# Expert loop of a mixture-of-experts stage: experts written out, counts read one expert ahead, and a tile's rows taken later

## The reference, cut to what matters

```python
x = attention(q, k, v, beta)              # (3072, 384), a delta-rule scan
x = leaky_relu(x @ moe_w_in) @ moe_w_out  # (3072, 384), dense
do_compute = x @ w_skip > 0               # rows that fail this are copied
e_idx, gate_w = best of 8 experts by softmax(x @ w_gate)
for e in range(8):
    rows = do_compute & (e_idx == e)
    h = maximum(x[rows] @ w1[e], 0)             # 384 -> 1024
    out[rows] = x[rows] + gate_w * (h @ w2[e])  # 1024 -> 384
```

## Time and profile before

| | |
|---|---|
| median of 3 runs | 902.17 us (901.98 to 902.83) |
| the profiled execution | 900.34 us |
| its span, first to last instruction | 898.6 us |
| granted TensorE clock, mean | 0.968 |
| PE busy | 776.0 us, 86% |
| DVE busy | 662.2 us, 74% |
| ACT busy | 496.4 us, 55% |
| POOL busy | 414.3 us, 46% |

### The profile page before, as it was taken

One profiled execution on the slowest core, in us unless ns is written; L12 is line 12 of the kernel. 1 busy time (PEld: TensorE's weight loads), 2 busy tenths in 40 slices (PEclk: granted clock), 3 DMA queues, 4 the chain that ended last, 5 costly groups with the idle time before them and its releaser, 6 DMA issues.

```text
span 898.6 us, 27698 instructions
## 1 busy us (share of the span) xinstructions
PE 776.0 (86%) x10782; PEld 625.4 (70%) x10783; DVE 662.2 (74%) x1334; ACT 496.4 (55%) x1108; POOL 414.3 (46%) x498
## 2 busy tenths in 40 slices
PE   0122679999999999999999999999999899999996
PEld 0122558787778787777878788878777777778774
DVE  6655978888887988887888887876768873563382
ACT  5426456767666666667676756554455651441261
POOL 5104153636354544535362724352352665564463
PEclk9995589999999999999999999999999999999998
DMA  9599177687687686868667686347416765263100
GB/s 214 148 233 163 28 116 123 133 140 143 116 149 133 120 162 113 133 124 138 127 121 149 114 144 121 77 71 231 169 30 200 246 230 188 70 214 120 44 16 16
DMA packets 357277, 119.76 MB, mean 133 GB/s; under 512 B 330450, under 2 KB 348420, under 8 KB 356784
## 3 DMA queue, kind: packets, MB, share of 16 engines
q1 hardware_dynamic: 351424, 104.33, 55.7%
q0 software_dynamic: 3232, 7.64, 2.5%
q10 hardware_dynamic: 2512, 6.29, 2.0%
HBM read 63.53 MB, written 21.25 MB: 94 GB/s over the span
## 4 chain that ended last, share of the span: by engine, by line
PE 37%; DVE 20%; issue 10%; SPq 10%; DMA 8%; ACT 8%; POOL 5%; DVEq 0%; POOLq 0%; ACTq 0%
PE b_h L743 8%; PE b_acc L756 8%; PE b_acc L849 7%; PE b_h L836 6%; DVE stage L1483 3%; PE b_ch L682 3%; SPq L442 2%; DVE inv L1409 2%; SPq L498 2%; ACT operands L954 2%; DMA operands<-operands 2%; SPq L510 2%; DVE inv L1415 2%; DMA operands<-nq 1%; PE b_gr L644 1%
## 5 line engine op out<-in xcount | busy, mean ns | idle before, releaser
L1908 POOL TENSOR_TENSOR stage<-stage 128x256 f16<-128x256 f32 x192 | 143.4, 747 | 246.9 <-ACT stage L954 246.0
L743 PE MATMUL b_h<-stage,wt 128*128 128x256 f16 x1728 | 221.8, 274 | 6.7 <-DVE stage L1342 6.3
L756 PE MATMUL b_acc<-wt,stage 128*128 128x384 f16 x1152 | 218.4, 326 | 3.7 <-POOL stage L1908 2.8
L743 PEld LDWEIGHTS b_h<-stage,wt 128*128 128x128 f16 x1728 | 159.1, 98 | 27.3 <-DVE stage L1342 8.2
L756 PEld LDWEIGHTS b_acc<-wt,stage 128*128 128x128 f16 x1152 | 106.7, 97 | 58.2 <-POOL stage L1908 5.7
L954 ACT ACTIVATE stage<-stage 128x256 f16<-128x256 f32 x192 | 80.0, 417 | 108.7 <-DVE stage L1483 107.8
L1483 DVE SCALAR_TENSOR_TENSOR stage<-b_h,stage 128x256 f32<-128x256 f32 x192 | 80.7, 420 | 42.1 <-ACT stage L1074 40.4
L849 PE MATMUL b_acc<-wt,operands 128*128 128x384 f16 x552 | 98.9, 330 | 7.1 <-DVE operands L1523 7.1
L836 PEld LDWEIGHTS b_h<-y,wt 128*128 128x128 f16 x1656 | 93.5, 98 | 6.5 <-issue 4.6
L836 PE MATMUL b_h<-y,wt 128*128 128x128 f16 x1656 | 96.5, 219 | 1.5 <-DVE y L1342 0.7
L1415 DVE TENSOR_REDUCE inv<-inv 128x30 f32<-128x90 f32 (+4 forms) x180 | 84.9, 472 | 5.6
(11 more groups left out here) (215 smaller groups left out, 1293.3 us busy)
## 6 DMA issues: line engine op xcount, KB each, us to landing
operands<-in_moe_w_dram SPq DMA_DIRECT2D x18, 1536.0 KB, 7.9
a_sys<-a_dram SPq DMA_DIRECT2D x24, 256.0 KB, 4.4
kc<-operands SPq DMA_DIRECT2D x22, 256.0 KB, 4.3
natq<-in_q_dram SPq DMA_DIRECT2D x24, 192.0 KB, 4.1
raw_v<-in_v_dram SPq DMA_DIRECT2D x24, 192.0 KB, 4.2
stage<-y SPq DMA_DIRECT2D x96, 48.0 KB, 2.0
x_dram<-stage SPq DMA_DIRECT2D x24, 192.0 KB, 2.8
out_dram<-stage SPq DMA_DIRECT2D x24, 192.0 KB, 3.4
```

What stands on the lines that cost most here:

```text
L743: mm = pe.matmul(b_h[f % 2][:, 0:GT], wt[0][:, a, d * FF + f * P:d * FF + (f + 1) * P], xT[:, g % 2, b, d, :], start=(i == 0), stop=(i == ...
L756: mm = pe.matmul(b_acc[w][:, 0:DM], g16[:, f % 4, a, w * P:(w + 1) * P], wt[1][:, b, f * DM:(f + 1) * DM], start=(f == 0 and (a, b) == PAR ...
L1908: pool.tensor_tensor(g16[:, f % 4, LO, :], g32[:, f % 4, :], g16[:, f % 4, HI, :], ALU.subtract).then_inc(g_lo, 1)
```

## The change

On ACT and DVE the eight experts are written out one by one, without the loop over pairs and its `If`. The counts of expert e+1 are read after the first tile of expert e. On DVE `tile_out` of a tile moves from behind `tile_in` of the next to behind quarter 0 of the next tile, and quarter 3 moves ahead of `tile_in(t+1)`. A last `tile_out` stands at the end. On POOL the copy to `raw_v` becomes a step of its own (`keep`); from tile 3 on it stands ahead of `tile_next`. In `tile_back` two waits change places. PE and SP are as before.

```diff
@@ ScalarE @@
-            def expert(e, q, last=None):
-                n = act.value_load(tile_n[0:1, 0, ds(e, 1)], min_val=1, max_val=NT)
-                before = act.value_load(tile_n[0:1, 1, ds(e, 1)], min_val=0, max_val=FIRST + MAXT)
+            def counts(e):
+                return (act.value_load(tile_n[0:1, 0, ds(e, 1)], min_val=1, max_val=NT),
+                        act.value_load(tile_n[0:1, 1, ds(e, 1)], min_val=0, max_val=FIRST + MAXT))
+            n, before = counts(0)
+            for e in range(E):
                 act.wait_ge(eh_done, 1 + 2 * before)
                 act.sem_inc(act_waited, 1)
-                if last is None:
-                    tile(before, q)
-                else:
-                    with act.If(last < E // 2 - 1):
-                        tile(before, q)
-                    with act.If(last >= E // 2 - 1):
-                        tile(before)
+                tile(before, QUARTERS[e])
+                n_next, before_next = counts(min(e + 1, E - 1))
                 with act.If(n > 1):
                     with act.Fori(1, n) as j:
                         tile(before + j)
+                n, before = n_next, before_next
@@ VectorE @@
             tile_in(FIRST)
-            tile_out(3)
             split_lo(1, 1, 2, 2)
             def tile(t, q=(None, None, None, None)):
                 if q[0]:
                     split_lo(*q[0])
-                hidden_low(t, 0)
+                tile_out(t - 1)
                 if q[1]:
                     split_lo(*q[1])
-                hidden_low(t, 1)
+                hidden_low(t, 0)
                 if q[2]:
                     split_lo(*q[2])
-                tile_in(t + 1)
-                tile_out(t)
+                hidden_low(t, 1)
                 if q[3]:
                     split_lo(*q[3])
+                tile_in(t + 1)
...
+            n, before = counts(0)
+            for e in range(E):
+                tile(before, QUARTERS[e])
+                n_next, before_next = counts(min(e + 1, E - 1))
                 with dve.If(n > 1):
                     with dve.Fori(1, n) as j:
                         tile(before + j)
+                if e < E - 1:
+                    n, before = n_next, before_next
+            tile_out(before + (n - 1))
@@ GpSimd @@
-            def tile_back(t):
+            def keep(t):
                 pool.wait_ge(yo_ready, 1 + t)
                 waited()
                 pool.tensor_copy(xg_keep[:], tiles[:, ds(t % RING, 1), :].rearrange("p a m -> p (a m)")
                                  ).then_inc(xg_kept, 1)
+
+            def tile_back(t):
                 pool.wait_ge(yo_scattered, 16 * t + 16)
                 pool.sem_inc(yo_left, 1)
                 pool.tensor_copy(id_out[:], ids[:, ds(t, 1)]).then_inc(ids_ready, 1)
+                pool.wait_ge(ids_ready, 2 * t + 3)
+                waited()
                 pool.wait_ge(yo_ready, 1 + t + 1)
-                waited()
-                pool.wait_ge(ids_ready, 2 * t + 3)
                 waited()
...
-                tile_next(t)
+                if t < FIRST - 1:
+                    tile_next(t)
+                    keep(t)
+                else:
+                    keep(t)
+                    tile_next(t)
...
             with pool.Fori(FIRST, total) as t:
+                keep(t)
                 tile_next(t)
                 tile_back(t)
```

More of the change, by code:

```diff
@@ L1307, in _ @@
             act.wait_ge(tiles_ready, 1)
-            def expert(e, q, last=None):
-                n = act.value_load(tile_n[0:1, 0, ds(e, 1)], min_val=1, max_val=NT)
-                before = act.value_load(tile_n[0:1, 1, ds(e, 1)], min_val=0, max_val=FIRST + MAXT)
+            def counts(e):
+                return (act.value_load(tile_n[0:1, 0, ds(e, 1)], min_val=1, max_val=NT),
+                        act.value_load(tile_n[0:1, 1, ds(e, 1)], min_val=0, max_val=FIRST + MAXT))
+            QUARTERS = [((1, 1, 2, 3), None, (2, 0, 1, 0), (2, 0, 1, 1)), (None, (2, 0, 1, 2), None, (2, 0, 1, 3))]
+            QUARTERS += [[(e + 1, 1 - e % 2, e % 2, i) for i in range(4)] for e in range(2, E - 1)]
+            QUARTERS += [(None, None, None, None)]
+            n, before = counts(0)
+            for e in range(E):
                 act.wait_ge(eh_done, 1 + 2 * before)
                 act.sem_inc(act_waited, 1)
-                if last is None:
-                    tile(before, q)
-                else:
-                    with act.If(last < E // 2 - 1):
-                        tile(before, q)
-                    with act.If(last >= E // 2 - 1):
-                        tile(before)
+                tile(before, QUARTERS[e])
+                n_next, before_next = counts(min(e + 1, E - 1))
                 with act.If(n > 1):
@@ L1833, in tile, with counts @@
                     split_lo(*q[0])
-                hidden_low(t, 0)
+                tile_out(t - 1)
                 if q[1]:
                     split_lo(*q[1])
-                hidden_low(t, 1)
+                hidden_low(t, 0)
                 if q[2]:
                     split_lo(*q[2])
-                tile_in(t + 1)
-                tile_out(t)
+                hidden_low(t, 1)
                 if q[3]:
                     split_lo(*q[3])
[L1845 to L1854, removed]
+                tile_in(t + 1)
+            def counts(e):
+                return (dve.value_load(tile_n[0:1, 0, ds(e, 1)], min_val=1, max_val=NT),
+                        dve.value_load(tile_n[0:1, 1, ds(e, 1)], min_val=FIRST, max_val=FIRST + MAXT))
+            QUARTERS = [((1, 1, 2, 3), None, (2, 0, 1, 0), (2, 0, 1, 1)), (None, (2, 0, 1, 2), None, (2, 0, 1, 3))]
+            QUARTERS += [[(e + 1, 1 - e % 2, e % 2, i) for i in range(4)] for e in range(2, E - 1)]
+            QUARTERS += [(None, None, None, None)]
+            n, before = counts(0)
+            for e in range(E):
+                tile(before, QUARTERS[e])
+                n_next, before_next = counts(min(e + 1, E - 1))
                 with dve.If(n > 1):
```

## The result

The changed kernel takes 908.60 us in the median of 7 runs (905.65 to 912.88). The kernel before took 901.98 in the median of 7 beside it (899.37 to 902.89). The ratio is 1.0087, with a 95% interval of 1.0061 to 1.0113: slower by some 8 us (the two medians lie 6.6 apart). The profiled execution took 912.88, the longest of the seven, and the profiled one of before 900.34. So the two traces lie 12.5 us apart, more than half as much again as typical runs do.

A forecast was written before the change was run, and what follows sets the result against it. From 680 us on the kernel was taken as PE work with stalls in and behind weight-splitting tiles. Losses of 2.05 + 1.9 + 0.1 = 4.05 us put the profiled run at 904.4 and the median at 906.2, range 899.3 to 910.0.

The forecast's parts named there:

- the sum: Whole kernel: losses of 2.05 in quarter tiles, 1.9 by gathers and 0.1 in tile 4, together 4.05 us slower.
- Quarter tiles: Tiles that split weights: 9.14 us of DVE work ahead of the next tile bounds them; together 2.05 us lost.
- the written-out code: ACT and DVE programs: more instructions might fetch slower; taken as zero cost, at most 0.72 us.
- POOL's order: Copy to `raw_v` delays the copy to `natk` by 0.50 us; hidden in tiles without quarters.
- One more copy ahead of `natk`, 0.3: Full quarter tiles: POOL's extra copy ahead of `natk` costs PE about 0.3 us each (0 to 0.8).
- The gather behind a quarter tile: Tiles 7, 12 and 14: gathers start later and rows land late; 1.9 us lost (gain 0.6 to loss 5).
- the slower landing: Gather behind a quarter tile: landing slower by 1.3 us makes a stall of 1.9 us instead of 0.6.
- Tile 4: Earlier low half against a later gather for tile 5: 0.1 us lost, bounds gain 2.9 and loss 1.9.
- The level of the clock: Tile 4: after PE idles 2 to 3 us, tile 5 starts at 722.5 at full clock, up to 725.7 at lower.
- The inference that descriptors are written beside a DVE instruction with two SBUF inputs: Skill page's rule, doubted by the prediction; by it tile 4's issue ends some 0.8 us sooner, sum 0.8 less.
- A (faster): Rival: gathers land in time, clock stays, tile 4 gains 2.9; 2.75 us less, 899.4; chance 0.25.
- C (the gathers decide): Rival: three gathers behind weight loads cost 1.9 each, tile 4 its 1.9; 9 us slower, 911; chance 0.10.

The follow-up runs named there:

- e1: Kernel before with only experts written out and counts read one expert ahead on ACT and DVE, DVE's tile order and POOL untouched: ratio 0.9984 to the kernel before.
- e3: Kernel before with only POOL's order changed, `keep` ahead of `tile_next`: ratio 1.0015 to the kernel before.
- e5: Changed kernel with POOL's part undone, the kept copy again behind the gather: ratio 1.0084 to the kernel before.
- e9: Changed kernel with the weight loads of experts 2 to 7 bringing only an eighth of their columns: ratio 1.0013 to the kernel before.
- e12: Changed kernel with DVE's tile order as before the change and the second weight matrix's loads held back until gathered rows landed: ratio 0.9975 to the kernel before.

## Why the prediction was right, and where its sizes were off

The direction, the mechanism and the places were right; the size of one term was not. The median, 908.60, is in the stated range but just above the forecast's own 904.0 to 908.5: the loss is 6.6 us by the medians and 7.9 by the ratio, where the sum had 4.05. By the profile, of a long run, tiles 4 to 22 lost 10.5. By the steps of the prediction:

- *Quarter tiles.* Forecast: about 9.9 for tiles 11, 13 and 10.2 for 20, 10.5 for 6 and 21. Measured: 9.70, 9.89, 10.37, 10.39, 10.06. Together they lost 1.43, forecast 2.05. The 9.14 us of DVE work in a row took 9.17 in tile 11, started 0.23 after the up stage (forecast 0.3); tile 20 had 9.18 and 0.22. Tile 13 came out at its 9.9 by luck: quarter 0 started 0.43 ahead of the up stage, but one quarter took 2.72 instead of 1.75, and the row was 10.18 long. In tiles 6 and 21 it started 0.92 and 0.58 after the up stage (forecast 1.1). That the written-out code costs nothing was shown by e1, and POOL's order as a small thing by e3 and e5.
- *One more copy ahead of `natk`, 0.3.* The transposes waited 0.40 for it in tile 11 and, by the same timeline, in tiles 6, 20 and 21; without POOL's part (e5) tiles 6, 11 and 20 are 0.17 to 0.45 faster, but tile 21 is 0.41 slower.
- *The gather behind a quarter tile.* This is the mis-sized term, and by the runs nearly the whole loss: with the small loads (e9) 1.2 us of the 7.9 are left, and by its trace the quarter tiles' loss is made up by a faster tile 4. Forecast 1.9 for tiles 7, 12 and 14 together, measured 6.89. The place of the gather was right: 0.90 after the up stage in tiles 7 and 12 (forecast 0.8). The landing was put at 6.1 after the up stage and `natk` at 6.6; in tile 7 `natk` ended at 8.3 (755.27 - 746.98), in tile 12 at 7.6. The forecast took 4.3 from the issue's end to the landing; with the second matrix's load issued just ahead it was 5.8 in tile 7 and 5.1 in tile 12. That is about the slower landing that the prediction had bounded with 1.9 for each gather. The transposes waited 2.20, 1.49 and 0.88, 4.57 together. In tile 7 the clock fell as well, and its second down half took 3.79, some 1.7 more than at full clock, which no term of the sum held.
- *Tile 4.* Forecast a loss of 0.1, with a bound of 1.9 to the bad side; measured 1.83. Its rows in the changed kernel:

```profile
712.80 3.41 DVE L1338 SCALAR_TENSOR_TENSOR stage<-operands,stage 128x1536 f16<-128x1536 f32 x2
...
712.93 1.65 POOL L1943 COPY id_in<-spare 128x1 uint32<-128x1 uint32 x1 [0.17 <-POOL operands L1952]
...
715.44 1.69 POOL L1926 DMA_INDIRECT natq<-x_dram,id_in  x1 [0.85 <-POOL id_in L1943]
...
716.35 0.37 SPq L544 DMA_DIRECT2D operands<-in_moe_w_dram  x1
716.66 0.68 DVE L1519 SCALAR_TENSOR_TENSOR operands<-b_h,operands 128x512 f16<-128x512 f32 x1
...
720.13 1.78 POOL L2022 COPY raw_v<-operands 128x385 f32 x1
...
722.41 0.51 POOL L1951 COPY natk<-natq 128x384 f32<-128x384 f32 x1 [0.50 <-DMA natq<-x_dram,id_in]
```

The times after the up stage (713.18; 711.29 in the forecast) are nearly the forecast's. The copy of the row numbers got in between the two quarters and ended 1.40 after it (forecast 1.6). The gather's issue ended 3.95 after it (4.3), with SP's load of 716.35 beside it. The low half came 3.5 after it (4.0). `natk` was done 9.7 after it (8.7 to 9.6). The forecast gave all of this to the landing. But POOL's kept copy (L2022) ended only at 721.91, half a us ahead of `natk`: a quick landing would have gained that half us and no more, and e9 shows the same. The level of the clock had been left open. It fell: the second down half took 4.05 and the next up stage 4.68, some 2.4 together above the usual times. So the tile ended at the forecast's bad end, 14.32 (14.4).

The inference that descriptors are written beside a DVE instruction with two SBUF inputs, which the prediction weighed against the trace (the Trainium skill, SBUF — State Buffer, Who interferes with whom; the page names `tensor_tensor`, the instruction here is a `scalar_tensor_tensor`), fails here too: the issue at 715.44 took 1.69 with a quarter running at its start, against 1.05 for the ones alone.

Of the rivals, A (faster) fell just where it was said to decide: tile 4 took over 11 us. C (the gathers decide) is nearer to the profiled run than the forecast is, and the median of the runs lies between the two. What stays open is how the gathers vary from run to run: the changed kernel's seven runs spread over 7.2 us, those of before over 3.5, and only one of each was traced. The traced run is 4.3 us above the median, about what the low clock took in it (4.1); whether the typical run kept its clock is not shown. If it did, the terms for the gathers and tile 4 are less wrong for it than for the trace. The median is in the stated range because that range was drawn most of the way to C. That e5 and e12 moved tile 21 and tile 20 by half a us either way was not followed up.

## What to carry to other kernels

When work is moved on one engine, follow the small transfers that its neighbour issues behind it, and look what large transfer stands just ahead of them: here the rows of a gather (128 rows of 385 floats, 197 KB) were copied 6.9 us after its issue began behind a load of 1.5 MB, and 3.8 us behind a load of an eighth of that. Look also at the copies on the neighbour itself: in tile 4 they kept PE waiting 2.90 us even where the transfer was quick. A wait that holds the large load back until the small one has landed can give back most of such a loss (6.0 of 7.9 us here). And an issue by GpSimd is work on GpSimd: placed ahead of copies that PE needs, it cost more than the late transfer it was to cure.

## What the runs showed of the hardware that I had not expected

- The rows of a gather behind a full weight load were copied 6.88 us after its issue began, behind one of an eighth of the size 3.76 us after, at the same place in the tile.
- The granted clock did not follow the length of PE's wait alone. It fell after waits of 2.20 and 3.45 us in the changed kernel and of 2.38 in the kernel before, but not after 2.90 in the kernel with small loads, whose next 12 matmuls took the usual 2.11 and whose next window has the full clock:

```profile
725.54 0.55 PE L829 MATMUL b_tr<-ident,natk 128*128 128x128 f32 x3 [2.90 <-POOL natk L1953]
...
725.93 2.11 PE L851 MATMUL b_acc<-wt,operands 128*128 128x384 f16 x12
...
726.00:728.00 2.00, 2.00 (x15) 1.13 (x14) 0.56 (x1) 0.82 (x2) 0.94 (x2) 1.00 0.36 105
```

- The program's untouched first part began its last stage at 673.5 to 679.6 us, by kernel. A comparison of two traces by their ends alone would have taken up to 6 us of that for an effect of the edit.
